# Block attention, convolution gate and gated MLP on one core: GpSimd's add of v's rows is moved to the head of a pair, with three edits to the order around it

## The reference

```python
# 1. attention, q, k, v: (2 batches, 8 heads, 768 positions, 64)
k_sum = k.reshape(B, H, 24, 32, 64).max(axis=3)      # per block of 32 keys
v_sum = v.reshape(B, H, 24, 32, 64).mean(axis=3)
scores_l = q @ k^T / 8, kept where |i - j| < 16      # a band of near keys
scores_s = q @ k_sum^T / 8 + log(32)                 # 24 block keys
a = softmax(concat(scores_l, scores_s))
x = a @ concat(v, v_sum)                             # -> (2, 768, 512)
# 2. gate by a causal convolution of 5 taps per channel
gate = sigmoid(sum_k conv_w[k] * x[s - 4 + k])
x = (gate * (x @ w_val)) @ w_out
# 3. gated MLP
u, v = split(relu(x @ w_in))                         # 512 + 512 columns
v = layer_norm(v); v = w_spatial @ v + b_spatial     # along positions
out = (u * v) @ w_out2                               # -> (2, 768, 512)
```

## Time and profile before

| What | Value |
|---|---|
| median of 3 runs | 319.25 us (318.87 to 321.8) |
| the profiled execution | 319.96 us |
| its span, first to last instruction | 318.2 us |
| TensorE busy | 294.8 us (93%) |
| VectorE busy | 174.8 us (55%) |
| ScalarE busy | 150.7 us (47%) |
| GpSimd busy | 123.5 us (39%) |
| mean granted TensorE clock | 0.995 |

### The profile page before, as it was taken

One profiled execution on the slowest core, in us unless ns is written; L12 is line 12 of the kernel. 1 busy time (PEld: TensorE's weight loads), 2 busy tenths in 40 slices (PEclk: granted clock), 3 DMA queues, 4 the chain that ended last, 5 costly groups with the idle time before them and its releaser, 6 DMA issues.

```text
span 318.2 us, 5354 instructions
## 1 busy us (share of the span) xinstructions
PE 294.8 (93%) x1768; PEld 269.7 (85%) x1768; DVE 174.8 (55%) x579; ACT 150.7 (47%) x463; POOL 123.5 (39%) x140
## 2 busy tenths in 40 slices
PE   6789797788779998899999999999999999999996
PEld 6689697778768997878899999888899999988885
DVE  6869887797666999995210001878765333320000
ACT  3669797797787576635212223443433111122212
POOL 6422755866653669534000000343458332320000
PEclk9979999999999999999999999999999999999999
DMA  7999976785250053200000000211101000002222
GB/s 158 230 215 219 221 161 169 185 207 125 53 171 34 21 164 99 82 0 3 0 0 2 0 0 2 99 49 35 43 24 35 0 0 2 0 1 101 99 99 99
DMA packets 51801, 25.52 MB, mean 80 GB/s; under 512 B 44586, under 2 KB 46910, under 8 KB 51774
## 3 DMA queue, kind: packets, MB, share of 16 engines
q1 hardware_dynamic: 51774, 25.18, 31.3%
HBM read 22.03 MB, written 3.15 MB: 79 GB/s over the span
## 4 chain that ended last, share of the span: by engine, by line
PE 72%; DVE 7%; issue 6%; ACT 6%; SPq 5%; DMA 2%; POOL 1%; DVEq 0%; ACTq 0%
PE psum L681 56%; PE psum L633 4%; DVE psum L1045 4%; PE psum L618 3%; PE psum L604 3%; ACT probs L825 2%; PE psum L645 2%; PE psum L569 2%; SPq L373 2%; DMA k_nat<-in_k_dram 1%; PE psum L777 1%; DVE work L1106 1%; DVE gate L1045 1%; SPq L360 1%; SPq L372 1%
## 5 line engine op out<-in xcount | busy, mean ns | idle before, releaser
L516 POOL TENSOR_TENSOR g_lo<-work,g_hi 128x384 fp32r<-128x384 f32 x32 | 32.3, 1024 | 35.8 <-ACT g_hi L952 26.2
L516 POOL TENSOR_TENSOR vn_lo<-work,vn_hi 128x512 fp32r<-128x512 f32 x12 | 15.5, 1293 | 72.9 <-DVE vn_hi L1143 72.9
L825 ACT ACTIVATE probs<-neg_s,neg_max 128x120 f32<-128x120 f32 x96 | 36.7, 387 | 1.5 <-DVE neg_max L971 1.5
L971 DVE CUSTOM_DVE_ANT_0 neg_s<-psum,mask 128x120 f32<-128x120 f32 x96 | 24.7, 277 | 14.1 <-PE psum L604 14.0
L633 PE MATMUL psum<-probsT,v_win 120*128 120x128 f32 x192 | 30.3, 281 | 0.0
L604 PE MATMUL psum<-k_win,qT 128*128 128x120 f32 x192 | 29.6, 277 | 0.7 <-DVE qT L1009 0.7
L1045 DVE SCALAR_TENSOR_TENSOR psum<-xT,conv_c,psum 128x384 f32<-128x384 f32 x48 | 26.0, 617 | 3.3 <-ACT psum L867 3.3
L604 PEld LDWEIGHTS psum<-k_win,qT 128*128 128x128 f32 x192 | 25.7, 194 | 1.0 <-issue 0.9
L633 PEld LDWEIGHTS psum<-probsT,v_win 120*128 120x128 f32 x192 | 25.7, 194 | 0.3
L839 ACT ACTIVATE probsT<-psum 120x256 f32<-120x256 f32 x48 | 18.1, 378 | 15.9 <-PE psum L618 15.5
L1121 DVE TENSOR_TENSOR wsp_lo<-psum,wsp_hi 128x384 fp32r<-128x384 f32 x12 | 6.6, 549 | 33.3 <-ACT wsp_hi L933 33.3
(11 more groups left out here) (125 smaller groups left out, 725.9 us busy)
## 6 DMA issues: line engine op xcount, KB each, us to landing
v_win<-in_v_dram SPq DMA_DIRECT2D x16, 240.0 KB, 3.0
k_nat<-in_k_dram SPq DMA_DIRECT2D x16, 192.0 KB, 4.5
v_nat<-in_v_dram SPq DMA_DIRECT2D x8, 384.0 KB, 4.8
out_dram<-work SPq DMA_DIRECT2D x11, 256.0 KB, 2.0
q_nat<-in_q_dram SPq DMA_DIRECT2D x14, 192.0 KB, 3.6
raw<-in_moe_w_spatial_dram SPq DMA_DIRECT2D x6, 384.0 KB, 3.1
raw<-in_moe_w_out_dram SPq DMA_DIRECT2D x8, 256.0 KB, 2.7
raw<-in_moe_w_in_dram SPq DMA_DIRECT2D x8, 256.0 KB, 3.0
```

The costliest lines, as they stand in the source:

```text
L516: nc.gpsimd.tensor_tensor(dst_lo, src, dst_hi.bitcast(F32), ALU.subtract).then_inc(lo_sem, 1)
L825: ins = nc.scalar.activation(probs[:, i % RING, g, :], neg_s[:, i % 3, g, :], ACT.Exp, bias=neg_max[:, i % 4, g:g + 1], scale=-1.0, accum_ ...
L971: nc.vector.tensor_tensor_reduce(out=neg_s[:, i % 3, g, :], in0=bank_s(i)[:, g, :], in1=mask[:, e, :], scale=-(float(D) ** -0.5), scalar=B ...
```

## The change

GpSimd adds the rows of v for the next pair (`add_v(p + 1)`) as the first thing in pairs 1 to 6, ahead of `split_x`, where it stood behind `k_tails`; pair 0 keeps its order. The wait in `spread_means` counts accordingly. TensorE scores steps 0 and 1 on the first piece of q, before the other two pieces of q and the convolution weights are turned, and VectorE masks these two steps before it copies those pieces. ScalarE does single half first taps at steps 48, 49, 52 and 53 (channels 0 and 1) where it did both halves of channel 0 at step 50. VectorE's list of drain taps grows by three taps in each of the last two drain steps. The load of w_out's third piece (piece 6) moves from pair 7 to pair 6.

```diff
@@ spread_means(p), GpSimd
-                    pool.wait_ge(v_nat_added, p + 1)
+                    pool.wait_ge(v_nat_added, 2 * p + 1)
@@ GpSimd's loop over pairs
             for p in range(PAIRS):
+                if 1 <= p < PAIRS - 1:
+                    add_v(p + 1)
                 if p >= 2:
                     split_x(p - 2)
                 spread_means(p)
                 if p + 1 < PAIRS:
                     k_tails(p + 1)
-                    add_v(p + 1)
+                if p == 0:
+                    add_v(1)
@@ TensorE, ahead of its loop over steps
             turn_q(0, 0)
+            scores(0)
+            scores(1)
+            for piece in range(1, PIECES):
+                turn_q(0, piece)
+            pe.wait_ge(conv_loaded, 16)
+            nc.tensor.transpose(bank_x(0)[:, 0, 0:TAPS * C], conv_raw[:, :],
+                                ident[0:TAPS * C, 0:TAPS * C]).then_inc(conv_turned, 1)
@@ TensorE's loop (the same turns after scores(0) are taken out)
-                if i < STEPS:
+                if 2 <= i < STEPS:
                     scores(i)
@@ ScalarE's loop
                 if i in FIRST_AT:
-                    for half in range(2):
-                        first_tap(FIRST_AT.index(i), half)
+                    first_tap(*divmod(FIRST_AT.index(i), 2))
@@ ScalarE, between
-                    if len(FIRST_AT) <= n + 1 < B * C:
+                    if len(FIRST_AT) // 2 <= n + 1 < B * C:
@@ VectorE, ahead of its loop (which then masks from step 2 on)
-            for piece in range(PIECES):
+            turned_q(0, 0)
+            dve.wait_ge(mask_step, MASK_STEPS)
+            for i in range(2):
+                for g in range(2):
+                    mask_scores(i, g)
+            for piece in range(1, PIECES):
                 turned_q(0, piece)
-            dve.wait_ge(mask_step, MASK_STEPS)
@@ constants
-PIECES_OF = ((), (), (0,), (1,), (2,), (3,), (4, 5), (6, 7))
+PIECES_OF = ((), (), (0,), (1,), (2,), (3,), (4, 5, 6), (7,))
-DRAIN_TAPS = (0, 0, 0, 2, 2, 2, 0, 0)
-FIRST_AT = (50,)
+DRAIN_TAPS = (0, 0, 0, 2, 2, 2, 3, 3)
+FIRST_AT = (48, 49, 52, 53)
```

## The result

The changed kernel takes 309.09 us (median; 307.91 to 310.84) against 319.06 us (318.34 to 321.8) for the kernel before on the same chip: ratio 0.9677, 95% interval 0.9603 to 0.975, or 10.0 us less. Its profiled execution took 309.19 us (span 307.5).

The account below looks back on a forecast made before the run. TensorE bounds the stretch from 138.24 us; ahead of it, its six waits for GpSimd's add recur pair after pair. Terms 8.7 - 0.4 + 0 + 0.3 + 0 = 8.6 us off 319.25 give 310.7 us, range 308.0 to 313.8.

Parts of the forecast that it names:

- The add: GpSimd's add moved to the pair's head: TensorE's six waits before `means` (line 645) go, 8.7 us gained, less 0.4 for hand-offs.
- hand-offs: Between three nearly equally busy engines in a pair: 0.07 us lost on each of five pairs, -0.4 us, bounds 0 and 2.4.
- rival B: ScalarE and VectorE take over as the bound of a pair: 2.4 us lost instead of 0.4, time 312.7 us; chance 0.14.
- v's landing: At the pair's head on GpSimd: v lands before the add needs it, 0.3 us to spare at the median, none at slowest.
- the first pair the tightest: v for pair 2, issued at 16.64, lands at 21.4 to 23.4 us: cost 0, or up to 0.5 with the slowest landing.
- rival F: The add at the pair's head waits for v's landing, delaying GpSimd's later work; a 9.6 us landing gives 322.5 us; chance 0.03.
- The early scores: At the start, two steps scored on q's first piece: 0 us, between -0.3 and +0.3, since all ends in load waits.
- w_out's piece: In the last pair, piece 6 issued earlier: its 1.69 us wait goes, piece 7 waits 1.5; gain 0.3 us, 0 to 1.07.
- rival C: w_out's piece 7 queues behind v and lands after 4.8 us, not 2.7: 2.1 us late, time 312.8 us; chance 0.08.
- Taps: First and drain taps: leads of 1.0 and 1.4 us used up by w_in's fourth piece; 0 us, between -1.0 and +1.4.
- Rival D: Both small edits, w_out's piece and taps, give 1.07 and 1.4 us instead of 0.3 and 0: 308.5 us; chance 0.12.

## Why the prediction was right, and which term was off

**The add, forecast 8.7 - 0.4.** Mechanism right, shown from three sides: alone it gives the whole gain, everything else alone gives none, and shortening the add in its old place by 0.76 us shortens the gap by 0.76. The step that failed is "Without the gap a pair takes 11.21 - 1.66 = 9.55 us", and with it the 0.07 us put on each for hand-offs. With the add alone moved a pair takes 9.31 us, so a gap of 1.66 cost 1.90 us; the short add, whose gap of 0.90 cost 1.14, gives the same difference of 0.24. Over five pairs that is 1.2 us gained, outside the bounds of 0 to 2.4 lost that the text gave the term. It can be read in TensorE's rows, here those of before:

```profile
59.06 0.38 PE L569 MATMUL psum<-ident,q_nat 128*128 128x128 f32 x2
61.10 0.89 PE L645 MATMUL psum<-v_nat,sel 128*120 128x128 f32 x6 [1.66 <-issue]
61.83 0.38 PE L618 MATMUL psum<-ident,probs 128*120 128x128 f32 x2
```

The last two matmuls ahead of the gap run their 0.38 us to the end (59.06 to 59.44, where the wait begins), whereas in after `means` follows 0.22 us behind such a pair (64.05 to 64.27); and what follows `means` starts 0.73 us behind it after a gap (61.10 to 61.83) and 0.66 without (64.27 to 64.93). 0.16 and 0.07 make 0.23. So a gap here costs its idle time and 0.23 us around it; that these are the emptying and refilling of TensorE's pipeline is my reading, and no run separates it. What I took for ScalarE's 9.38 and VectorE's 9.59 us of own time held short waits as well (they are busy 9.23 and 9.07); both fit into 9.31, so rival B is out. Five pairs give 9.5 us with the add alone, where 7.9 was forecast for them (5 x 1.66 less 0.4). In after's own trace it is 8.66, because of the next point.

**v's landing, forecast as covered.** Here the text set itself a mark: v's landing showing up as what GpSimd waits for would fail the forecast. It did show up, 0.7 to 5.6 us in every pair, and the step "v is there by 60.8 to 63.3" with the add ending at 63.9 was wrong. The landings came as forecast (4.5 to 6.7 us in after); what was off is when GpSimd asks. The text let GpSimd be free at 62.9, 6.4 us after the issue at 56.49, as in a pair of 11.21 us that still ends with an add. In after it is free 3.0 to 3.9 us after the issue for the last four of these adds (58.05, by the row above, against an issue at 54.20). Nor was the first pair the tightest: one pair later GpSimd is free at 25.92, ahead of the issue at 26.62, and that is the wait that reached TensorE.

GpSimd's slack took nearly all of these waits. They cost TensorE 0.92 us in one pair of this execution. Of the seven traces with after's order of v's loads and the add moved, four have such a wait, of 0.42 to 1.70 us, and three (the add alone, no tap edits, w_out as before) have none; nor have the two with v issued early. So rival F's mechanism is real, and one order of issues away. That the run with v issued behind its window rows ends at 324.27 us, close to the 322.5 that F was priced at, is chance: F priced a landing 9.6 us after the issue, whereas there v lands 3.4 to 5.6 us after an issue that comes late. That F's price is one for one was too simple: after the longest waits TensorE also ran at half its clock.

**The early scores, forecast 0.** Right. The 1.30 us that the first stretch lost is the gap at pair 2 (0.34) and, for most of the rest, the half-clock stretch that this execution did not have, and that the one without the edit did not have either. In the four kernels with the add moved and v in after's order whose clock stayed up there, `means` of pair 2 starts at 25.92 to 26.18 us, in the three others at 27.20 to 28.85.

**w_out's piece, forecast 0.3 (0 to 1.07).** The wait moved to the fourth piece as said (1.22 us; forecast 1.5), and what piece 7 queues behind did not make it late: it landed 2.98 us after its issue, so rival C, and with it what the Trainium skill's "DMA: Bandwidth & Descriptors", section Queues, rings and completion order, would have made of it, did not come. But the comparison was made with the wrong wait: I took the v loads to need SyncE 4.3 us "as now", and with the add moved they need 3.0, so without the edit only 0.4 to 0.8 us of wait are left. In the run with all but the add's move the edit did shorten the wait (1.1 for 1.69). Beside the add's move it is worth 0, or -0.4 (53.90 against 53.55 us).

**Taps, forecast 0.** Right, and by the way described. The timelines of VectorE, ScalarE and GpSimd in after:

```profile
88.59 1.39 DVE L1048 SCALAR_TENSOR_TENSOR psum<-xT,conv_c,psum 128x384 f32<-128x384 f32 x2 [0.18 <-ACT psum L871]
91.47 0.43 DVE L1019 COPY xT<-psum 64x256 f32<-64x256 f32 x1 [1.49 <-PE psum L636]
...
96.81 0.83 POOL L502 CAST x_hi<-xT 128x768 fp32r<-128x768 f32 x1 [5.88 <-ACT xT L852]
...
103.42 0.63 ACT L837 ACTIVATE win_u_hi<-raw 128x512 fp32r<-128x512 f32 x1 [1.64 <-DMA raw<-in_moe_w_in_dram]
...
105.37 2.00 POOL L516 TENSOR_TENSOR g_lo<-work,g_hi 128x384 fp32r<-128x384 f32 x2
...
106.54 0.56 DVE L1113 SCALAR_TENSOR_TENSOR work<-gate,psum 128x384 f32<-128x384 f32 x1 [1.14 <-PE psum L691]
```

Taps early (15.0 us after pair 7's `means`, before 18.3), an idle 1.49 us before the tile copy, GpSimd's last split late, w_in's fourth piece late, and VectorE's fourth product waiting. The last row names TensorE, but by the program that product needs the buffer that the first `g_lo` frees, and the first of the two `g_lo` ends at about 106.4. The two kernels that take w_in's parts ahead of that split confirm it: with the wait gone 0.93 and 0.94 us come through. With the add alone, and so the taps as before, the way from channel 1's taps to the products took 31.02 us (96.30 to 127.32), in after 31.96: what the taps gained was lost on that way. Rival D needed it free.

In sum: 8.3 forecast for the add against 10.2 measured with it alone, 0.3 against 0 for the rest. By stretches, ahead of pair 2, in the five pairs and behind them, the forecast was 0.3, 7.9 and 0.3; the trace with the add alone has 0.28, 9.48 and 1.16 less than before, that of after 1.30, 8.66 and 0.81. The five pairs hold 1.6 more than forecast, as 5 x (9.62 - 9.31) = 1.55 says, and v's landing took back 0.9 in after. Behind them the add's move shortened the wait for w_out's piece by itself (1.69 to 0.39), a gain that the forecast gave to another edit and put at 0.3. The 1.0 us beyond forecast ahead of pair 2 is luck of after's execution, the clock. So the total came out near, 10.0 for 8.6, with the main term too small and errors of either sign beside it; with 2 to 3 us between runs of one kernel the medians can't part them further.

## What to carry to other kernels

A gap of an engine that is otherwise full can cost more than the idle time shown (here 1.90 for 1.66): take the pair's length without a gap from its instructions' spacing in an undisturbed stretch, not from length less idle time. When an instruction moves ahead in one engine's order, work out the time from its inputs' issue to their landing in the new, shorter period; cover that holds at the old pace may be gone at the new one, and the order of issues on the loading queue decided here between a gain of 10 us and a loss of 4. Small edits priced against waits of the old schedule should be priced again on the schedule that the large edit leaves.

## What was not expected of the hardware

- Twelve of the traces have the same wait of 2.56 to 2.62 us for `add_v(1)` ahead of 18 us. From 18 to 21 us TensorE's granted clock was 0.50 to 0.65 in seven of them and 1.00 in five, with kernels with and without the early scores on either side. It was 0.52 in before, after 2.17 us, and 1.00 with the short add, after 1.71. It went with up to 2.4 us more between the `means` of pairs 1 and 2; how much of the spread of 2 to 3 us between runs it makes is not shown. What decides it stays open.
- In the run with v issued behind its window rows, the clock fell to about 0.5 after waits of 3.01 and 3.69 us and stayed at 1.00 after one of 1.14; but it fell to 0.55 (30.09 to 32.00 us) after one of 1.03 us, which began 1.6 us behind one of 0.99.
- The same issue on SyncE (line 373, a load of v's window rows, 16 times) took 0.3 to 2.0 us in before, with a median of 0.56, and 0.3 to 2.8 in after, with a median of 1.08; what stands behind it on that queue is issued later by it. The DMA share in a pair is 1.10 in after and was 0.71; that the one makes the other was not tried.
